# Local softmax by ScalarE's biased exponentials, a new order of each attention step on all engines, an earlier split of w_out

## What is computed

```python
def attention(q, k, v):          # 4 batches, 8 heads, 576 positions, 64 wide
    # down-sampled: q, k, v averaged over groups of 4 positions, full softmax, result repeated 4 times
    # local: softmax of the scores with |i - j| < 4 only
    return out_up + out_local
x = attn_out.transpose(0, 2, 1, 3).reshape(2304, 512)
x = ((x @ w1) * (x @ w2) @ w3) @ w_out        # d_ff 1024
h = x @ w_in                                  # d_ff 2048
out = (h * sigmoid(h)) @ w_out2
```

## Time and profile before

| | |
|---|---|
| median of 3 runs | 831.73 us (831.5 to 831.91) |
| the profiled execution: time, span | 833.47 us, 831.7 us |
| busy: TensorE, VectorE, ScalarE, POOL | 796.8, 606.3, 319.0, 285.5 us |
| chain that ended last, by engine | PE 87%, ACT 4%, DVE 3%, POOL 3%, issue 2% |
| TensorE busy tenths, first eight of 40 slices | 5 7 8 9 9 8 8 9, then 9 |
| granted clock, tenths, first eight of 40 slices | 8 7 8 9 9 9 9 9 |

### The profile page before, as it was taken

How to read it: one execution, slowest core, us unless ns; L and a number is a source line. 1 busy time by engine, 2 the same in 40 slices (tenths; PEclk the granted TensorE clock), 3 DMA queues, 4 the chain that set the end, 5 groups by cost and what they waited for, 6 DMA issues and landing times.

```text
span 831.7 us, 13580 instructions
## 1 busy us (share of the span) xinstructions
PE 796.8 (96%) x5336; PEld 712.7 (86%) x5336; DVE 606.3 (73%) x948; ACT 319.0 (38%) x581; POOL 285.5 (34%) x343
## 2 busy tenths in 40 slices
PE   5789988999999999999999999999999999999998
PEld 4567766789999999999999988988888988888886
DVE  5668888886667876767769867759867769856644
ACT  2445455632244333522235432344432344432321
POOL 6767788543233223142332212212312312311100
PEclk8789999999999999999999999999999999999999
DMA  7545754211101110111013213112412212412102
GB/s 258 199 147 154 246 170 124 64 52 51 50 27 52 51 50 28 51 52 51 29 48 103 76 51 93 59 52 76 152 52 80 73 51 71 158 50 76 51 1 76
DMA packets 23039, 69.81 MB, mean 84 GB/s; under 512 B 2496, under 2 KB 2496, under 8 KB 22976
## 3 DMA queue, kind: packets, MB, share of 16 engines
q1 hardware_dynamic: 22832, 68.36, 25.7%
q10 hardware_dynamic: 144, 0.59, 0.2%
HBM read 64.23 MB, written 4.72 MB: 83 GB/s over the span
## 4 chain that ended last, share of the span: by engine, by line
PE 87%; ACT 4%; DVE 3%; POOL 3%; issue 2%; POOLq 0%; DVEq 0%; ACTq 0%
PE ps L977 41%; PE ps L1035 24%; PE ps L1006 12%; PE ps L1059 4%; ACT prob_d L455 2%; PE ps L1078 1%; PE ps L1112 1%; PE ps L1137 1%; PE ps L1121 1%; POOL prob L383 1%; POOL prob_d L392 1%; PE ps L1104 1%; DVE x L748 1%; ACT w3t L417 1%; DVE wa L665 1%
## 5 line engine op out<-in xcount | busy, mean ns | idle before, releaser
L977 PE MATMUL ps<-xb,wa 128*128 128x384 f32 x2016 | 405.3, 338 | 2.0 <-DVE a L805 1.4
L977 PEld LDWEIGHTS ps<-xb,wa 128*128 128x128 f32 x2016 | 355.0, 188 | 24.5 <-DVE a L805 2.1
L348 POOL TENSOR_TENSOR rw<-rw 128x256 f32<-128x256 f32 x48 | 43.4, 904 | 441.1 <-DMA rw<-in_sets 336.6
L805 DVE TENSOR_TENSOR mu<-ps,mu 128x384 f32<-128x384 f32 x132 | 73.2, 554 | 122.1 <-PE ps L977 121.9
L1006 PE MATMUL ps<-g,r 128*128 128x512 f32 (+1 forms) x576 | 124.9, 338 | 1.6 <-issue 1.6
L1035 PE MATMUL ps<-w2h_even,g 128*128 128x512 f32 x432 | 113.2, 394 | 0.0
L1035 PE MATMUL ps<-w2h_odd,g 128*128 128x512 f32 x432 | 112.5, 393 | 0.0
L559 ACT ACTIVATE a<-a 128x384 f32<-128x384 f32 x72 | 37.9, 526 | 189.1 <-DVE a L805 189.1
L665 DVE TENSOR_TENSOR wa<-rw,wa 128x1024 fp32r<-128x1024 f32 x96 | 107.3, 1119 | 2.9 <-ACT wa L417 2.6
L1006 PEld LDWEIGHTS ps<-g,r 128*128 128x128 f32 x576 | 97.7, 188 | 10.1 <-issue 2.2
L1035 PEld LDWEIGHTS ps<-w2h_odd,g 128*128 128x128 f32 x432 | 79.9, 188 | 11.9
(11 more groups left out here) (78 smaller groups left out, 809.8 us busy)
## 6 DMA issues: line engine op xcount, KB each, us to landing
rw<-in_sets SPq DMA_DIRECT2D x48, 512.0 KB, 3.5
w2r<-in_w_out SPq DMA_DIRECT2D x24, 512.0 KB, 3.5
qk<-in_qk SPq DMA_DIRECT2D x15, 576.0 KB, 5.5
vg<-in_vg SPq DMA_DIRECT2D x16, 336.0 KB, 5.9
vw<-in_vw SPq DMA_DIRECT2D x16, 320.0 KB, 3.2
out<-osb SPq DMA_DIRECT2D x18, 256.0 KB, 2.3
wn<-in_w SPq DMA_DIRECT2D x16, 256.0 KB, 5.3
raw<-in_w_out SPq DMA_DIRECT2D x2, 1024.0 KB, 8.8
```

Source lines behind the costliest of these rows:

```text
L348: nc.gpsimd.tensor_tensor(blocks[:, 4, :], blocks[:, 0, :], blocks[:, 1, :], ALU.add).then_inc(s1_ready, 1)
L805: nc.vector.tensor_tensor(o, half_bank(k, i), term, ALU.add).then_inc(sum_ready, 1)
L977: e = nc.tensor.matmul(ps[:, (k + i) % 2, 0:TH], wa[:, k % 2, l, A_SLOT[i], a * P:(a + 1) * P], xb[:, i, r, a, :], start=(i in (0, 1, 4) a ...
```

## The change

- The mask is added with the opposite sign: two VectorE instructions (one per head) compute mask - score/8, the row minimum replaces the maximum, and ScalarE takes ten exponentials of 64 columns with that minimum as bias, scale -1 and the sum in `tot`. POOL's subtraction and VectorE's sum go.
- `w3_low` moves from VectorE to POOL (between the two normalisations), the high half of a finished fold and `take_down` from ScalarE to VectorE.
- TensorE's order: both scores, turn local, fold parts 0 to 2, turn down, fold part 3, weighted down-sampled sum, weighted local sum. In step 1 it has twelve transposes of the identity (`warm`) after the local scores.
- ScalarE: high half of w3 first, then copies and exponentials in two portions; POOL: pooled values first. VectorE computes pair 1's mask already in step 0.
- w_out: both halves are loaded in SyncE's turn 1, cast in steps 1 and 2, subtracted one step later (even blocks VectorE, odd ones POOL).
- Weight sums come one quarter a step from step 9, first token sums every second step; first tokens' and weights' high and low halves come partly in steps 13 to 15. A small exponential on ScalarE stands at the start. `summed` becomes two semaphores.

The diff, cut to its core (in the order SyncE, POOL, ScalarE, VectorE, TensorE):

```diff
+        gate = sb("gate", [1, 2])
...
+        W_OUT = {1: (0, 1, 2, 3), 2: (4, 5, 6, 7)}
...
             load_qk(0)
             load_vg(0)
+            load_vw(0)
             for t in range(PAIRS):
...
+                if t == 1:
+                    load_w_out(0)
                 if t >= FOLD - 2:
                     load_w3(t - FOLD + 2)
-                if t in (FOLD - 2, FOLD - 1):
-                    load_w_out(t - FOLD + 2)
+                if t == 1:
+                    load_w_out(1)
...
-            def sums(k, half):
+            def weight_sum(k, i):
...
+            def w3_low(q):
+                pool.wait_ge(w3_hi, q + 1)
+                m4 = slice(4 * (q % 2), 4 * (q % 2) + 4)
+                nc.gpsimd.tensor_tensor(w3t[:, 1, m4, :].rearrange("p m c -> p (m c)"), wn[:, q % 2, :],
+                                        w3t[:, 0, m4, :].rearrange("p m c -> p (m c)").bitcast(F32),
+                                        ALU.subtract).then_inc(w3_lo, 1)
...
-                if s == 0:
-                    pool_values()
-                pool.wait_ge(max_l, s + 1)
-                nc.gpsimd.tensor_tensor(pr, pr, low[:, u, :, None].broadcast_to([P, 10, BW]), ALU.subtract
-                                        ).then_inc(shifted, 1)
-                if s > 0:
-                    pool_values()
+                pool_values()
+                for n in W_OUT.get(s - 1, ())[1::2]:
+                    pool.wait_ge(r3_hi, n + 1)
+                    nc.gpsimd.tensor_tensor(r3[:, n, 1, :], raw3[:, n, BANK:], r3[:, n, 0, :].bitcast(F32),
+                                            ALU.subtract).then_inc(r3_lo_pool, 1)
+                if s >= AHEAD:
+                    weight_sum((s - AHEAD) // 4, (s - AHEAD) % 4)
                 pool.wait_ge(inv_l, s + 1)
                 nc.gpsimd.tensor_tensor(pr, pr, inv[:, u, :, None].broadcast_to([P, 10, BW]), ALU.mult
                                         ).then_inc(norm_l, 1)
+                for q in splits_of(s + 1):
+                    if q < HALVES - 1:
+                        w3_low(q)
                 pool.wait_ge(inv_d, s + 1)
...
+            act.wait_ge(consts, 1)
+            nc.scalar.activation(gate[:, 0:1], ident[0:1, 0:1], ACT.Exp)
...
-                def exps_local():
-                    act.wait_ge(shifted, s + 1)
-                    pr = prob[:, u, :, :, :].rearrange("p g h k -> p (g h k)")
-                    nc.scalar.activation(pr, pr, ACT.Exp, scale=D ** -0.5).then_inc(exp_l, 1)
+                def exps_local(groups):
+                    act.wait_ge(low_l, s + 1)
+                    for g in groups:
+                        for h in range(2):
+                            pr, n = prob[:, u, g, h, :], 2 * g + h
+                            e = nc.scalar.activation(pr, pr, ACT.Exp, bias=low[:, u, n:n + 1], scale=-1.0,
+                                                     accum_out=tot[:, u, n:n + 1])
+                    if NG - 1 in groups:
+                        e.then_inc(exp_l, 1)
...
                 for q in splits_of(s):
                     w3_high(q)
+                if s == 0:
+                    exps_local(range(NG))
+                    act.wait_ge(blank, 2)
+                elif s == 1:
+                    exps_local(range(LATE))
+                    copy_pt()
+                    copy_ptd()
+                    exps_local(range(LATE, NG))
+                else:
+                    copy_pt()
+                    exps_local(range(LATE))
+                    copy_ptd()
+                    exps_local(range(LATE, NG))
                 exps_down()
+                for n in W_OUT.get(s, ()):
+                    act.wait_ge(r3_in[n // (MT // 2)], 16)
+                    copy_act(r3[:, n, 0, :], raw3[:, n, BANK:]).then_inc(r3_hi, 1)
+                if s in (PAIRS - 3, PAIRS - 2):
+                    first_weights_high(s - PAIRS + 3)
+                if s == PAIRS - 1:
+                    act.wait_ge(scored, 2 * PAIRS)
+                    act.wait_ge(pooled, PAIRS)
+                    tokens_high(0, 0)
+                    tokens_high(0, 1)
...
             def take_w3o(m):
+                dve.wait_ge(w3_mul, 2 * m + 2)
+                nc.vector.tensor_copy(r2[:, m, 0, :], ps[:, fold_bank(2 * m), :]).then_inc(w3o_hi, 1)
...
+            def mask_local(s):
...
+                for h in range(2):
+                    e = nc.vector.scalar_tensor_tensor(prob[:, u, :, h, :],
+                                                       ps[:, pS + h, 0:NG * BW].rearrange("p (g k) -> p g k", g=NG),
+                                                       -D ** -0.5, mask[:, :, :], ALU.mult, ALU.add)
+                e.then_inc(masked, 1)
+                dve.wait_ge(masked, s + 1)
+                nc.vector.tensor_reduce(low[:, u, :].rearrange("p (g h) -> p g h", h=2), prob[:, u, :, :, :],
+                                        AX.X, ALU.min).then_inc(low_l, 1)
...
-                mask_local()
-                if s + 1 < PAIRS:
-                    pool_pair(s + 1)
-                max_down()
-                sum_local()
-                for q in splits_of(s):
-                    w3_low(q)
+                if s != 1:
+                    mask_local(s)
                 if s > 0:
-                    take_local(0)
-                    take_local(1)
-                sum_down()
+                    max_down()
+                    if s + 1 < PAIRS:
+                        pool_pair(s + 1)
+                else:
+                    pool_pair(1)
+                    max_down()
+                    mask_local(1)
+                for n in W_OUT.get(s - 1, ())[0::2]:
...
                 for q in halves_of(s):
                     if q % 2 == 1:
                         take_w3o(q // 2)
-                if s in (FOLD - 1, FOLD):
-                    w_out_low(s - FOLD + 1)
-                if AHEAD <= s < AHEAD + 4:
+                if AHEAD <= s and (s - AHEAD) % 2 == 0:
                     dve.wait_ge(x_ready, 2 * 2 * HP)
-                    token_sum(0, s - AHEAD)
+                    token_sum(0, (s - AHEAD) // 2)
+                totals_local()
+                if s == PAIRS - 1:
+                    tokens_low(0, 0)
+                    weights_low(0, 0)
+                if s > 0:
+                    take_down()
+                    take_local(0)
+                    take_local(1)
+                totals_down()
...
                 if s == PAIRS:
-                    for part in range(4):
+                    for part in range(2):
                         multiply(HALVES - 3, part)
                     turn_local()
+                    multiply(HALVES - 3, 2)
                     turn_down()
-                    for part in range(3):
+                    multiply(HALVES - 3, 3)
+                    for part in range(4):
                         multiply(HALVES - 2, part)
-                    weighted_local_waits()
-                    multiply(HALVES - 2, 3)
+                    weighted_down()
                     weighted_local()
-                    weighted_down()
...
                 scores_local()
-                for q in qs:
-                    multiply(q, 0)
+                if s == 1:
+                    warm(12)
+                scores_down()
                 if s > 0:
                     turn_local()
-                scores_down()
-                for q in qs:
-                    multiply(q, 1)
+                for part in range(3):
+                    for q in qs:
+                        multiply(q, part)
                 if s > 0:
                     turn_down()
-                    weighted_local_waits()
-                    for q in qs:
-                        multiply(q, 2)
-                    weighted_local()
-                    weighted_down()
                 for q in qs:
                     multiply(q, 3)
+                if s > 0:
+                    weighted_down()
+                    weighted_local()
```

182 lines of the change are left out of this document (60 added, 122 removed).

## The result

| | before | changed |
|---|---|---|
| median of the runs | 831.82 us (4 runs, 831.5 to 833.74) | 824.42 us (4 runs, 822.8 to 824.51) |
| profiled execution: time, span | 833.47, 831.7 us | 824.40, 822.6 us |
| first MLP matmul | 165.61 us | 155.99 us |

A forecast was written before the change was run, and what follows sets the result against it. Only the 165.6 us attention part could move, bounded by TensorE's work and waits. 48.0 + 86.4 + 14.2 = 148.6 saves 17.0: profiled 816.5, median 814.7 us, range 811 to 819.

The forecast's parts named there:

- The last step: Final attention step: 14.2 us instead of 11.34, with a new 2.85 us wait for turn_down, bounds 0 and 3.5.
- Steps 0 to 4: First attention steps: step 5 begins at 48.0 us instead of 58.16, 10.2 us gained, bounds 7 and 12.
- The plain steps: Eleven steps from step 5: 7.85 us each instead of 8.74, 86.4 us in all, bounds 7.6 and 8.15 each.
- The base: Whole kernel: median 814.7 from profiled 816.5, since the earlier profiled execution stood 1.74 us above its median.
- my signs of being right: Pieces near 0.29 us, steps of 7.8, no L682 or L758 waits, MLP near 148.6, one last-step wait near 3 us.
- cover: Loads of w3 blocks: issued 1.3 us into a step, landing in 5.3, needed at 8.3, about 1.7 us spare.
- The rule: POOL and VectorE: two-port or two-SBUF-input VectorE instructions and SBUF-reading POOL ones exclude each other; 1.26 us per moved w3_low.
- rival (1): Plain steps: POOL and VectorE block each other, 8.35 us a step, 5.5 us back, 820.2 us; chance 0.17.
- Rival (3): Local exponentials don't overlap their reads: 0.567 us a piece, 10.2 us a step, slower at 840.6 us; chance 0.05.
- Rival (2): First steps win little, by low clock or late w_out: gain 4 instead of 10.2, 820.9 us; chance 0.12.
- a sign of being wrong: POOL's norm awaited every step, pitch over 0.33 us, granted clock 0.5 past 35 us, or MLPs over 666 us.
- Rival (4): Plain steps: TensorE stays at 8.74 us as another wait follows the fold's, 824.5 us; chance 0.06.

The follow-up runs named there:

- c0: The changed kernel itself, run again without an edit: 824.40 us, ratio to before 0.9911.
- e1: Changed kernel with VectorE's low halves of the first tokens and weights moved from step 15 to step 16, behind take_local: 824.73 us.
- e10: Changed kernel with VectorE's first token and weight low halves in step 16 and the last two blocks' w3_low moved from POOL to VectorE: 820.30 us.
- e7: Changed kernel with the casts and subtractions of w_out one step later, loads as changed: 838.59 us.
- e5: Changed kernel with w3_low of all steps back on VectorE, for the last two blocks in step 16: 822.92 us.
- e2: Changed kernel with ScalarE's two token copies in its last step moved behind w3_high of block 14: 827.21 us.

## Why the prediction was wrong

On the axis of the profiled executions the sum said 816.5 and 824.4 came. The 7.9 us between are 2.6 in the last step, 3.4 in steps 0 to 4, 1.4 in the eleven plain steps and 0.5 in the MLP part; with 1.7 for the base they make the 9.7 between 814.7 and the median of 824.42. By c0's profile (822.84) it is 4.5, 1.6, 0.4 and -0.1. The last step is the one term that lies outside its bounds in both. Step by step:

- **The last step: 16.75 us, and 18.66 in c0, not 14.2 (at most 14.8 by its bounds).** This is the step that failed. I costed only ScalarE's copies and POOL behind them. The change also puts tokens_low(0, 0) on VectorE ahead of take_local. It waits for that very copy, and turn local waits for take_local. I had the code of it in the diff and no term for it. The wait I did forecast, 2.85 us for turn down, was 0.40 (1.00 in c0). That one wait near 3 us stood in the last step, as my signs of being right said, is luck: it was another instruction, waiting for another engine. I also had POOL's w3_low and norm at their lengths alone, and no low clock behind a wait. In e1, without the first wait, w3_low takes 4.07 us and turn down waits 4.71. e10 removes both and gets 13.03.
- **Steps 0 to 4: step 5 at 51.4, not 48.0.** Up to step 3 the sum held within a microsecond: turn down of step 2 at 26.2 forecast, 26.00 measured, the end of step 3's local scores at 32.6 and 33.5. The rest is two things. POOL's pooled values took 2.58 us beside VectorE's w_out low halves, so turn local of step 4 came at 43.97 instead of 41.8; and the low clock that followed that wait cost the nine fold matmuls 1.4 us. In c0's profile, without this second stretch, step 5 begins at 49.55, though turn local of step 4 waits 2.34 us there. Of the bounds of this gain (7 to 12 us) the 6.8 measured is just outside and c0's 8.6 inside. The account of POOL here rests on the traces; no experiment takes it away.
- **The plain steps: 7.98 us, not 7.85.** The order and the loops were about right, the waits for L682 and L758 are gone, and steps 5 to 9 take 7.79 each, under the 7.85 that I took. The pieces have a pitch of 0.33, not 0.29; a linear cut from a 144-column row took off too much. 10 x 0.04 is 0.4 us on ScalarE, and the weighted sum waits 0.35 us, but both fit in the 7.79. The loss is all in steps 10 to 15. There POOL's weight sums and VectorE's token sums come in; four of them are 0.2 to 0.4 us longer, and step 11 takes 8.68: ScalarE waits for the w3 block, whose cover I had put at 1.7 us. It was issued at 93.10, behind a weight load, 2.8 us into its step and not 1.3, and was there 7.7 us later and not 5.3 (c0's step 11 takes 8.16). The eleven steps are inside their bounds (83.6 to 89.7 us).
- **The base: 1.7 us.** The sum is of absolute stretches, so it gives 816.5 for the changed kernel. I then took off the 1.74 us by which the profiled execution before stood above its median, as if the changed kernel inherited it. That execution had more low clock than most (a mean of 0.984; its faster neighbours have 0.993), the changed kernel's profiled one was at its own median (0.983). The kernel before spreads from 830.3 to 835.4 over all its runs, so a profile is one draw from a spread of that size. (A slip of mine in the mask, 0.98 us where 0.82 and 0.2 make 1.02, moves nothing.)
- **The rule.** The Trainium skill's exclusion of POOL and VectorE (SBUF — State Buffer, Who interferes with whom) was cited and given rival (1) with 0.5 us in each plain step. There it cost little: L736 has a mean of 0.304 us (0.234 before). It bit where several VectorE instructions with two SBUF inputs stand in a row, in steps 2, 3 and 16, as the 4.07 and 2.58 us show. So the two do exclude each other, but I had the place wrong, and the direction: I feared POOL holding up VectorE's short instructions, and what cost time was VectorE's row holding up POOL. Rival (1), 8.35 us a step, is out at 7.98.
- **The rivals.** Rival (3), slower, is out: a piece is 0.33 us, though that is just the value from which it would decide. Rival (2), little won in the first steps, is partly right: the clock was 0.50 again from about 45 to 48 us, which I had named as a sign of being wrong, and 6.8 us were won, between its 4 and my 10.2; e7 shows how much hangs on when w_out is split. Rival (4) gave 824.5 us, which is the time measured, and it is out all the same: other waits did come in place of the fold's, but a step is at 7.98 and not at 8.74. That its number fits is chance.

## To carry to other kernels

When a step is moved, write down for every engine what stands behind it in the queue, and follow the wait of the moved step to the producer's new place too; two moves that are each free (a copy to the end of ScalarE's step, its low half ahead of VectorE's output) can meet. In these traces a POOL instruction that reads SBUF beside a row of VectorE instructions with two SBUF inputs was done only after the row (4.07 us in e1, 3.24 in e5), so give such a row to a time when POOL's result isn't wanted, or keep both on one engine. And don't carry the distance of one profiled execution from its median over to the changed kernel: a sum of absolute stretches already gives the time, with the spread of single executions around it.

## What the runs showed of the hardware

- A 64-column exponential with a pointer bias and a sum takes 0.337 us and starts 0.33 us after the one before; the read of the sum (0.189 us) hides under the next. The estimate from the Trainium skill (ScalarE: Activation LUTs, What ACT_TABLE_LOAD costs) in the prediction was 0.24 without the read; its 280 ns + 0.833 ns a column without the overlap give an estimate of 0.333, near the duration of 0.337 measured. ScalarE's plain casts do overlap here: four of 0.630 us take 2.19 in a row, 0.11 less at each seam. That it is the read that takes the overlap from the exponentials isn't tried apart.
- POOL's subtraction of 512 columns took 1.28 us alone and 4.07 us beside three VectorE instructions in a row with two SBUF inputs each; it didn't get in between them and ended 1.12 us after the last. The other way round, VectorE's low half of 768 columns took 1.80 us beside that subtraction (e2), and 0.92 where POOL stood idle (e1, at 141.42).
- The same kernel at the same place has the granted clock of 0.50 in one execution and 1.00 in another, and executions of one kernel with a little more low clock were 1.5 to 2.4 us longer (c0). Some waits of TensorE of about 2 us and more in these traces are followed by a stretch at 0.50 and some aren't (a wait of 1.90 us in step 4 was, one of 2.34 in c0's wasn't), so a wait can cost more than its length: the nine fold matmuls behind the 1.90 us wait of step 4 took 3.73 us instead of 2.31. In the first 14 us the profile's clock reads 1.00 and isn't to be relied on: forty local scores take 1.34 us there (8.73 in the changed kernel) and 0.81 in the later steps (126.01 in the kernel before).
